# Turning the normalised softmax of a feed-forward: VectorE block transposes and DMA moves in place of TensorE transposes

## The chip, the cores and the metric

One NeuronCore of a Trainium2 chip runs the whole program. The metric is device time in microseconds. Three runs of the kernel before took 993.0, 997.02 and 998.18 us, with a median of 997.02 us.

## What is computed

The reference is a linear-attention recurrence over 768 time steps for 4 batches and 8 heads of 40 features, whose output is read as 3072 tokens of 320 features, followed by two feed-forward layers:

```python
h  = x @ w_in                                   # 320 -> 1024
sm = exp(h - max(h)) / (sum(exp(h - max(h))) + 1e-9)
solu = h * sm
ln = (solu - mean) / sqrt(var + 1e-6) * g_ln
x  = ln @ w_out                                 # 1024 -> 320
h2 = x @ w2_in                                  # 320 -> 2048
out = (max(h2, 0) + alpha * min(h2, 0)) @ w2_out  # 2048 -> 320
```

The change touches only the step between `ln` and `ln @ w_out` of the first feed-forward layer. The softmax, the mean and the variance run over the 1024 features of a token, so they are computed with tokens on the partitions; the product that follows contracts over the features, so its operand must have the features on the partitions. The normalised matrix is therefore turned (transposed) in between.

## The kernel before

**Stages.** The attention runs first, in 24 groups. The feed-forward is cut into 12 chunks of 256 tokens; a chunk has two tiles of 128 tokens (t = 0 and 1). Chunk 0's first layer runs beside the last attention groups. After that, `schedule` runs `step(c)` on each engine, c from 0 to 11 (steps 0 and 1 written out, steps 2 to 9 in a hardware loop over two at a time, steps 10 and 11 written out). Step c computes the second feed-forward layer of chunk c, and interleaved with it the first layer of chunk c + 1. So eleven of the twelve steps prepare a next chunk. Each engine runs its instructions strictly in the order in which the code lists them; semaphores connect the engines.

**TensorE in step c.** `layer1(c+1, 0)`, `layer2(c, 0)`, `layer1(c+1, 1)`, and then for q = 1 to 7 (each q is a pair of 128-feature blocks of the 2048) `layer2(c, q)` followed by `layer2_out(c, q-1)`. At q = 6, between the two, stand two calls of `turn_n`, one for each tile: 8 transposes of 128x128 each, from `soft[t]` into the PSUM tensor `bank`. After q = 7 come `layer1_out(c+1)`, which multiplies the turned matrix `nT` by `w_out` and needs both tiles (`nT_high`, `nT_low`), and `layer2_out(c, 7)`. All products are made of three matmuls of split operands: a high and a low part of each fp32 number.

**VectorE in step c.** `largest` (row maximum), `weigh` (the product h * sm), `normalise` (L1419, after a power that GpSimd computes) of chunk c + 1 are placed among the calls of `split(c, q)`, q = 0 to 7. `split` makes the rectified activation from `mid` and `slopes` (L1441), its high part (L1445) and its low part (L1368); `layer2_out(c, q)` on TensorE waits for it. `normalise(c+1, 0)` stands behind `split(c, 3)` and `normalise(c+1, 1)` behind `split(c, 4)`. `low_n` for both tiles (the low part of `nT`, L1368) stands behind `split(c, 6)`.

**ScalarE in step c.** `exponent` and `square` of chunk c + 1 among the calls of `rectify(c, q)` (L1278 and L1282), which make `slopes` from `mid`. `take_n` for both tiles (the high part of `nT`, rounded out of `bank`, L1222) stands behind `rectify(c, 6)`.

**SyncE in step c.** It issues all DMAs: three loads of x for chunk c + 2 (L1020), then it waits for `y_taken` and stores the output (L1087).

**Where a wait bites.** `layer2(c, q)` waits for `act_ready` of pair q - 2, `layer2_out(c, q)` waits for `act_low` of pair q. The buffer `stage2` (128x1024 fp32) serves as landing place for raw weights while step 0 runs, and is free after that. `soft[0]` and `soft[1]` are 128x1024 fp32 each.

Of the kernel before, what the change touches and what calls it, by code (L numbers as in the profile page):

```python
# [892 lines left out]
def feed_forward(nc, ctx, early, att, x_scr, wts, out):  # L893
# [53 lines left out]
    var_ready, rstd_ready, n_ready = sem("var_ready"), sem("rstd_ready"), sem("n_ready")  # L947
    nT_done, nT_high, nT_low = sem("nT_done"), sem("nT_high"), sem("nT_low")
    z_done, z_high, z_low = sem("z_done"), sem("z_high"), sem("z_low")
    z_part_ready, z_last_ready, z_last_high = sem("z_part_ready"), sem("z_last_ready"), sem("z_last_high")  # L950
# [37 lines left out]
    def wait_raw(eng, n):  # L988
        eng.wait_ge(raw_loaded[home[n]], 16 * len(held[n]) + 16)

    def bank(c, t):
        return banks[0 if isinstance(c, int) and c == 0 else t]
# [77 lines left out]
    def sync(sp):  # L1070
        sp.wait_ge(xT_low, 2)
        for n in range(7, len(pieces)):
            load_piece(sp, n)
        for saved in att["y_saved"]:
            sp.wait_ge(saved, NG // 2 * 16)
        sp.wait_ge(low_ready, len(pieces))

        def prologue():
            pass

        def step(c, k, nxt, far):
            if far:
                load_x(sp, c + 2, x_in[k])
            before = value(sp, c * 16)
            sp.wait_ge(y_taken, c * 2 + 2)
            wait(sp, y_saved, before)
            sp.dma_start(out[c], y_sb[:]).then_inc(y_saved, 16)  # L1087

        schedule(sp, prologue, step)
        sp.wait_ge(y_saved, NC * 16)  # L1090

    def tensor(pe):
# [6 lines left out]
        def layer1(c, t):  # L1099
# [8 lines left out]
            if isinstance(c, int) and c == 0 and t == 1:  # L1108
                pe.wait_ge(nT_high, 2)
                pe.wait_ge(nT_low, 1)  # L1110
# [11 lines left out]
        def turn_n(c, t):  # L1122

            pe.wait_ge(n_ready, 2 * c + t + 1)
            if isinstance(c, int) and c == 0 and t == 0:
                pe.wait_ge(small_loaded, 48)
# [5 lines left out]
        def layer1_out(c):  # L1132

            pe.wait_ge(nT_high, 4 * c + 4)
            pe.wait_ge(nT_low, 2 * c + 2)
# [64 lines left out]
        def step(c, k, nxt, far):  # L1200
# [5 lines left out]
            for q in range(1, PAIRS):  # L1206
                layer2(c, q)
                if nxt and q == 6:
                    for t in range(2):
                        turn_n(c + 1, t)  # L1210
                layer2_out(c, q - 1)
# [19 lines left out]
    def scalar(act):  # L1231
# [22 lines left out]
        def take_n(c, t):  # L1254

            if isinstance(c, int) and c == 0:
                act.wait_ge(att["rhs_done"], 21 + 2 * t)
            for half in range(2):
                act.wait_ge(nT_done, 4 * c + 2 * t + half + 1)
                high(act, nT[:, t, 0, half * 4:half * 4 + 4],  # L1260
                     bank(c, t)[:, half * 512:half * 512 + 512].rearrange("p (f t) -> p f t", f=4)).then_inc(nT_high, 1)

# [58 lines left out]
        def step(c, k, nxt, far):  # L1321
            if nxt:
                exponent(c + 1, 0)
            for q in range(PAIRS):
# [7 lines left out]
                if nxt and q == 3:  # L1332
                    square(c + 1, 1)
                if nxt and q == 6:
                    take_n(c + 1, 0)
                    take_n(c + 1, 1)
            if far:
# [38 lines left out]
    def vector(dve):  # L1376
# [45 lines left out]
        def low_n(c, t):  # L1422

            dve.wait_ge(nT_high, 4 * c + 2 * t + 2)
            if isinstance(c, int) and c == 0:
                dve.wait_ge(att["rhs_done"], 22 + 2 * t)
            low(dve, nT[:, t, 1], bank(c, t)[:].rearrange("p (f t) -> p f t", f=FT1), nT[:, t, 0]).then_inc(nT_low, 1)

# [69 lines left out]
        def step(c, k, nxt, far):  # L1498
            if nxt:
                largest(c + 1, 0)  # L1500
            for q in range(PAIRS):
# [9 lines left out]
                if nxt and q in (3, 4):  # L1511
                    normalise(c + 1, q - 3)
                if nxt and q == 6:
                    low_n(c + 1, 0)
                    low_n(c + 1, 1)
            if far:
# [112 lines left out]
```

## Time and profile before

| | value |
|---|---|
| median of three runs | 997.02 us (993.0 to 998.18) |
| profiled execution, first to last instruction (span) | 994.4 us |
| TensorE busy | 921.3 us, 93% of the span, 13248 matmuls |
| VectorE busy | 660.0 us, 66% |
| ScalarE busy | 437.6 us, 44% |
| GpSimd busy | 243.3 us, 24% |
| granted TensorE clock, mean | 0.972 |
| share of TensorE in the chain that ended last | 80% |

The page and the times give no total of the profiled execution's own beside its span; the median of the runs is 2.6 us above the span. The span has 31301 instructions. Busy time is an average over stages: the attention ends near 430 us, and the feed-forward's steps fill the rest. In a timeline a row tells the start in microseconds from the span's start, the duration, the engine, the line, the operation and what it writes and reads; what stands in brackets at its end is how long the engine was idle before it, and which instruction's end released it. "SPq" rows are DMA issues: the time that the sequencer spent on handing the transfer over, not the transfer. Successive instructions of one kind are merged into one row with a count.

### The profile page before, as it was taken

To read this page: it belongs to the slowest core of one execution; us is meant where nothing else is said; L and a number is where in the kernel's file an instruction comes from. 1 tells how busy PE (TensorE), PEld (TensorE's weight loads), DVE (VectorE), ACT (ScalarE), POOL (GpSimd) and SP (SyncE) were. 2 spreads that over 40 slices of the span, in tenths; PEclk is the share of its full clock that TensorE was granted. 3 is DMA by queue.
4 is the path that set the end of the run, shared out by engine and by line. 5 is a ranking of instruction groups with operands and counts; after the bars stand their busy time and mean duration, and the time that the engine had idled before them with its cause. 6 is when DMAs were issued, how large, how long until landed. Compare 5 with 4: busy or idle time off the path is not lost.

```text
span 994.4 us, 31301 instructions
## 1 busy us (share of the span) xinstructions
PE 921.3 (93%) x13248; PEld 874.5 (88%) x13248; DVE 660.0 (66%) x1135; ACT 437.6 (44%) x892; POOL 243.3 (24%) x453
## 2 busy tenths in 40 slices
PE   3378999999999989888999999999999999999997
PEld 3378989988999988887999999999999999999997
DVE  8967877878878655568565647575756656565734
ACT  3234444544545533346343535363434435353523
POOL 8676564765556550000000000000000000000000
PEclk9698999999999989989999999999999999999999
DMA  5725765557666542352011010000000000000000
GB/s 159 126 71 149 150 128 123 154 137 165 136 145 156 129 90 55 106 164 77 1 27 28 1 28 1 27 0 26 0 26 0 26 9 18 26 0 13 2 14 14
DMA packets 156813, 67.32 MB, mean 68 GB/s; under 512 B 120172, under 2 KB 146412, under 8 KB 156700
## 3 DMA queue, kind: packets, MB, share of 16 engines
q1 hardware_dynamic: 154588, 65.54, 27.6%
q8 instruction: 89, 1.46, 0.6%
q10 hardware_dynamic: 2112, 0.13, 0.2%
q14 instruction: 24, 0.20, 0.1%
HBM read 45.98 MB, written 19.66 MB: 66 GB/s over the span
## 4 chain that ended last, share of the span: by engine, by line
PE 80%; DVE 10%; issue 5%; ACT 3%; DMA 1%; POOL 1%; ACTq 0%; DVEq 0%; POOLq 0%
PE px L341 7%; PE acc L1095 6%; PE acc L1096 5%; PE acc L1097 5%; PE pq L402 5%; PE pa L310 4%; PE mid L1095 4%; PE mid L1096 4%; PE mid L1097 4%; PE bank L1095 3%; PE bank L1097 3%; PE bank L1096 3%; PE py L428 3%; PE pr L354 3%; PE pr L365 3%
## 5 line engine op out<-in xcount | busy, mean ns | idle before, releaser
L1354 POOL TENSOR_TENSOR stats<-stats 128x1 f32<-128x1 f32 x24 | 13.2, 549 | 552.8 <-DVE stats L1416 552.8
L1441 DVE SCALAR_TENSOR_TENSOR stage<-mid,slopes 128x512 f32<-128x512 f32 x96 | 66.4, 691 | 106.1 <-ACT slopes L1282 106.0
L1095 PE MATMUL acc<-wo_h,act_h 128*128 128x320 f32 x384 | 121.7, 317 | 8.4 <-DVE act_l L1368 7.7
L1278 ACT ACTIVATE stage<-mid 128x512 f32<-128x512 f32 x96 | 57.1, 595 | 160.2 <-PE mid L1166 160.2
L1096 PE MATMUL acc<-wo_h,act_l 128*128 128x320 f32 x384 | 118.5, 309 | 0.0
L1097 PE MATMUL acc<-wo_l,act_h 128*128 128x320 f32 x384 | 118.2, 308 | 0.0
L1095 PE MATMUL mid<-zT_h,w_h 128*128 128x256 f32 x384 | 107.9, 281 | 2.3 <-DVE zT_l L1368 2.3
L1096 PE MATMUL mid<-zT_h,w_l 128*128 128x256 f32 x384 | 107.5, 280 | 0.0
L1097 PE MATMUL mid<-zT_l,w_h 128*128 128x256 f32 x384 | 107.3, 279 | 0.0
L793 POOL TENSOR_TENSOR al<-al,prod 40x512 f32<-40x512 f32 x48 | 70.7, 1473 | 97.9 <-DMA al<-a_features_first 85.5
L1282 ACT ACTIVATE slopes<-stage,minus_alpha 128x256 f32<-128x256 f32 x192 | 87.3, 502 | 3.1
L1095 PEld LDWEIGHTS acc<-wo_h,act_h 128*128 128x128 f32 x384 | 72.2, 188 | 13.0 <-issue 11.0
L1095 PEld LDWEIGHTS mid<-zT_h,w_h 128*128 128x128 f32 x384 | 72.8, 190 | 3.5 <-DVE zT_l L1368 2.7
L1096 PEld LDWEIGHTS mid<-zT_h,w_l 128*128 128x128 f32 x384 | 72.8, 190 | 0.8
L1097 PEld LDWEIGHTS mid<-zT_l,w_h 128*128 128x128 f32 x384 | 72.9, 190 | 0.0
L1096 PEld LDWEIGHTS acc<-wo_h,act_l 128*128 128x128 f32 x384 | 72.4, 188 | 0.0
L1097 PEld LDWEIGHTS acc<-wo_l,act_h 128*128 128x128 f32 x384 | 72.2, 188 | 0.0
L310 PE MATMUL pa<-a_bd,wkb 128*128 128x128 f32 x336 | 54.8, 315 | 18.2 <-ACT a_bd L708 11.1
L1368 DVE TENSOR_TENSOR act_l<-stage,act_h 128x512 fp32r<-128x512 f32 x96 | 66.5, 692 | 3.3
L310 PEld LDWEIGHTS pa<-a_bd,wkb 128*128 128x128 f32 x336 | 46.9, 217 | 20.3 <-DMA masks<-masks_in 11.0
L816 POOL TENSOR_TENSOR s_x<-s_x,s_t 128x15 f32<-128x15 f32 (+4 forms) x165 | 61.3, 372 | 12.9
L1245 ACT ACTIVATE soft<-bank,stats 128x1024 f32<-128x1024 f32 x24 | 26.6, 1108 | 74.1 <-DVE stats L1399 74.1
(162 smaller groups left out, 2410.0 us busy)
## 6 DMA issues: line engine op xcount, KB each, us to landing
wkb<-wkb_features_first SPq DMA_DIRECT2D x46, 242.5 KB
rvu<-rv_features_first SPq DMA_DIRECT2D x48, 160.0 KB
l_scr<-lb SPq DMA_DIRECT2D x24, 256.0 KB, 4.4
x_scr<-x SPq DMA_DIRECT2D x24, 256.0 KB, 3.7
al<-a_features_first SPq DMA_DIRECT2D x48, 80.0 KB
sv<-v_time_first SPq DMA_DIRECT2D x48, 80.0 KB, 4.7
out<-y_sb SPq DMA_DIRECT2D x12, 320.0 KB, 2.2
d_scr<-s_x SPq DMA_DIRECT2D x12, 256.0 KB, 2.3
```

Source lines behind the costliest of these rows:

```text
L310: ins = pe.matmul(banks[:, h * P:(h + 1) * P], kbT[m % 3][:, h].rearrange("p a b -> p (a b)"), a_bd[:, :, h], start=True, stop=True)
L341: ins = pe.matmul(px[half * HALF:half * HALF + rows, h * T + first:(h + 1) * T], left, right, start=True, stop=True)
L402: ins = pe.matmul(pq[:, h * P:(h + 1) * P], vuT[m % 3][:, h].rearrange("p a b -> p (a b)"), rvu[m % 3][:, h, 0:4:3], start=True, stop=True)
L793: pool.tensor_tensor(al[m % 7][r, half], al[m % 7][r, half], prod[m % 9][r, :, 0:T], ALU.mult)\
L816: link(pool.tensor_tensor(tgt, tgt, s_t[:, 0:n_t, 0:n_j], ALU.subtract))
L1095: pe.matmul(o, left[0], right[0], start=start, stop=False)
L1096: pe.matmul(o, left[1], right[0], start=False, stop=False)
L1097: return pe.matmul(o, left[0], right[1], start=False, stop=stop)
L1278: act.activation(neg[q % 2][:], mid[q % 2][:], ACT.Relu, scale=-1.0).then_inc(neg_ready, 1)
L1282: act.activation(slope[q % 2][:, cols], neg[q % 2][:, cols], ACT.Copy, scale=minus_alpha[:, 2 * q + f:2 * q + f + 1]).then_inc(slope_ready, 1)
L1368: return dve.tensor_tensor(out_, in_, hi.bitcast(F32), ALU.subtract)
L1441: dve.scalar_tensor_tensor(out=act_f[q % 2][:], in0=mid[q % 2][:], scalar=0.0, in1=slope[q % 2][:], op0=ALU.max, op1=ALU.add).then_inc(act ...
```

## The change

From chunk 1 on, the turning of the normalised matrix takes another path; chunk 0 keeps the old one.

- TensorE no longer turns in the steps (the two calls of `turn_n` at q = 6 are gone).
- VectorE gets a `turn_n` of its own, right behind each `normalise`: one transpose instruction on 128x1024 fp32 that transposes every 32x32 block inside its own group of 32 partitions, from `soft[t]` into `turned` (the buffer `stage2`, one for both tiles). Before it, it waits on `n_moved` until the moves of the tile before have landed, since `turned` is single.
- SyncE gets `move_n`: per tile 16 DMAs, each of 32 partitions x 256 fp32 numbers (32 KB), which carry each block from `turned` to the partitions where it belongs, back into `soft[t]`. Each tile's 16 DMAs raise `n_moved` by 256. They stand behind the loads of x of the same step and in front of the store of the output.
- ScalarE's `take_n` is one instruction per tile in place of two, reads `soft[t]` in place of `bank`, and waits for `n_moved` of its tile. It moves from behind `rectify(c, 6)` (both tiles) to behind `rectify(c, 5)` (tile 0) and `rectify(c, 6)` (tile 1).
- VectorE's `low_n` reads `soft[t]` and moves likewise: behind `split(c, 5)` for tile 0 and behind `split(c, 6)` for tile 1.

```diff
--- before.py
+++ after.py
@@ -946,6 +946,7 @@
     soft_ready, mean_ready, square_ready = sem("soft_ready"), sem("mean_ready"), sem("square_ready")
     var_ready, rstd_ready, n_ready = sem("var_ready"), sem("rstd_ready"), sem("n_ready")
     nT_done, nT_high, nT_low = sem("nT_done"), sem("nT_high"), sem("nT_low")
+    tr_ready, n_moved = sem("tr_ready"), sem("n_moved")
     z_done, z_high, z_low = sem("z_done"), sem("z_high"), sem("z_low")
     z_part_ready, z_last_ready, z_last_high = sem("z_part_ready"), sem("z_last_ready"), sem("z_last_high")
     mid_done, act_ready, act_high, act_low = sem("mid_done"), sem("act_ready"), sem("act_high"), sem("act_low")
@@ -987,6 +988,18 @@
 
     def wait_raw(eng, n):
         eng.wait_ge(raw_loaded[home[n]], 16 * len(held[n]) + 16)
+
+    turned = stage2
+
+    def token_blocks(z):
+
+        return z.rearrange("p f (i t) -> p f i t", i=4)
+
+    def moved_n(c, t):
+
+        if isinstance(c, int) and c == 0:
+            return bank(c, t)[:].rearrange("p (f i t) -> p f i t", f=FT1, i=4)
+        return soft[t][:].rearrange("p (i f t) -> p f i t", i=4, f=FT1)
 
     def bank(c, t):
         return banks[0 if isinstance(c, int) and c == 0 else t]
@@ -1078,9 +1091,20 @@
         def prologue():
             pass
 
+        def move_n(c, t):
+
+            sp.wait_ge(tr_ready, 2 * c + t - 1)
+            for q in range(4):
+                for i in range(4):
+                    sp.dma_start(soft[t][32 * q:32 * q + 32, i * 256:i * 256 + 256],
+                                 turned[32 * i:32 * i + 32, q * 256:q * 256 + 256]).then_inc(n_moved, 16)
+
         def step(c, k, nxt, far):
             if far:
                 load_x(sp, c + 2, x_in[k])
+            if nxt:
+                for t in range(2):
+                    move_n(c + 1, t)
             before = value(sp, c * 16)
             sp.wait_ge(y_taken, c * 2 + 2)
             wait(sp, y_saved, before)
@@ -1106,7 +1130,7 @@
                 pe.wait_ge(w1_low, KT)
                 pe.wait_ge(att["kbn_ready"], 2 * NG)
             if isinstance(c, int) and c == 0 and t == 1:
-                pe.wait_ge(nT_high, 2)
+                pe.wait_ge(nT_high, 1)
                 pe.wait_ge(nT_low, 1)
             tok = slice(t * P, (t + 1) * P)
             for half in range(2):
@@ -1121,8 +1145,8 @@
 
         def turn_n(c, t):
 
-            pe.wait_ge(n_ready, 2 * c + t + 1)
-            if isinstance(c, int) and c == 0 and t == 0:
+            pe.wait_ge(n_ready, t + 1)
+            if t == 0:
                 pe.wait_ge(small_loaded, 48)
             for f in range(FT1):
                 ins = pe.transpose(bank(c, t)[:, f * P:(f + 1) * P], soft[t][:, f * P:(f + 1) * P], ident[:])
@@ -1131,7 +1155,7 @@
 
         def layer1_out(c):
 
-            pe.wait_ge(nT_high, 4 * c + 4)
+            pe.wait_ge(nT_high, 2 * c + 2)
             pe.wait_ge(nT_low, 2 * c + 2)
             def both(z):
                 return z.rearrange("p (t k) -> p t k", t=2)
@@ -1205,9 +1229,6 @@
                 layer1(c + 1, 1)
             for q in range(1, PAIRS):
                 layer2(c, q)
-                if nxt and q == 6:
-                    for t in range(2):
-                        turn_n(c + 1, t)
                 layer2_out(c, q - 1)
             if nxt:
                 layer1_out(c + 1)
@@ -1255,10 +1276,10 @@
 
             if isinstance(c, int) and c == 0:
                 act.wait_ge(att["rhs_done"], 21 + 2 * t)
-            for half in range(2):
-                act.wait_ge(nT_done, 4 * c + 2 * t + half + 1)
-                high(act, nT[:, t, 0, half * 4:half * 4 + 4],
-                     bank(c, t)[:, half * 512:half * 512 + 512].rearrange("p (f t) -> p f t", f=4)).then_inc(nT_high, 1)
+                act.wait_ge(nT_done, 2 * t + 2)
+            else:
+                act.wait_ge(n_moved, (2 * c + t - 1) * 256)
+            high(act, token_blocks(nT[:, t, 0]), moved_n(c, t)).then_inc(nT_high, 1)
 
         def take_z(c):
 
@@ -1331,9 +1352,8 @@
                     exponent(c + 1, 1)
                 if nxt and q == 3:
                     square(c + 1, 1)
-                if nxt and q == 6:
-                    take_n(c + 1, 0)
-                    take_n(c + 1, 1)
+                if nxt and q in (5, 6):
+                    take_n(c + 1, q - 5)
             if far:
                 take_x(act, c + 2, x_in[k])
             if nxt:
@@ -1421,10 +1441,17 @@
 
         def low_n(c, t):
 
-            dve.wait_ge(nT_high, 4 * c + 2 * t + 2)
+            dve.wait_ge(nT_high, 2 * c + t + 1)
             if isinstance(c, int) and c == 0:
                 dve.wait_ge(att["rhs_done"], 22 + 2 * t)
-            low(dve, nT[:, t, 1], bank(c, t)[:].rearrange("p (f t) -> p f t", f=FT1), nT[:, t, 0]).then_inc(nT_low, 1)
+            low(dve, token_blocks(nT[:, t, 1]), moved_n(c, t), token_blocks(nT[:, t, 0])).then_inc(nT_low, 1)
+
+        def turn_n(c, t):
+
+            dve.wait_ge(n_ready, 2 * c + t + 1)
+            wait(dve, n_moved, (2 * c + t - 2) * 256)
+            dve.transpose(turned[:].rearrange("p (q f t) -> p q f t", q=4, f=FT1),
+                          soft[t][:].rearrange("p (f q r) -> p q f r", q=4, f=FT1)).then_inc(tr_ready, 1)
 
         def low_z(c):
 
@@ -1510,9 +1537,9 @@
                     weigh(c + 1, 1)
                 if nxt and q in (3, 4):
                     normalise(c + 1, q - 3)
-                if nxt and q == 6:
-                    low_n(c + 1, 0)
-                    low_n(c + 1, 1)
+                    turn_n(c + 1, q - 3)
+                if nxt and q in (5, 6):
+                    low_n(c + 1, q - 5)
             if far:
                 low_x(dve, c + 2, x_in[k])
             if nxt:
```

## Rows read from the trace of the kernel before

**Rows 1.** Windows: stretch, length; busy of PE, PEld, DVE, ACT, POOL; clock; DMA; GB/s.

```profile
664.00:705.00 41.00, 40.72 (x298) 39.07 (x297) 24.65 (x46) 18.74 (x38) 0.55 (x1) 1.00 0.06 16
```

**Rows 2.** The waits, TensorE from 470 us on: total us, times, longest.

```profile
PE acc L1095 <- DVE act_l L1368: 6.4, 11, 1.8
```

**Rows 3.** The chain that ended last, from 440 us on, in one step.

```profile
663.65 1.75 PE bank L1128 x16
...
709.64 1.75 PE bank L1128 x16
...
716.73 1.84 PE bank L1142 x16
```

**Rows 4.** TensorE's timeline in that step.

```profile
705.89 0.31 PE L1095 MATMUL acc<-wo_h,act_h 128*128 128x320 f32 x1
...
707.65 0.28 PE L1095 MATMUL mid<-zT_h,w_h 128*128 128x256 f32 x1
...
709.47 1.91 PE L1128 MATMUL bank<-ident,soft 128*128 128x128 f32 x16
...
711.14 0.39 PE L1095 MATMUL acc<-wo_h,act_h 128*128 128x320 f32 x1
```

**Rows 5.** VectorE's timeline in the same step.

```profile
702.75 0.81 DVE L1419 TENSOR_SCALAR soft<-soft,stats 128x1024 f32<-128x1024 f32 x1 [0.66 <-POOL stats L1354]
...
703.73 0.69 DVE L1441 SCALAR_TENSOR_TENSOR stage<-mid,slopes 128x512 f32<-128x512 f32 x1 [0.17 <-ACT slopes L1282]
...
704.92 0.69 DVE L1368 TENSOR_TENSOR act_l<-stage,act_h 128x512 fp32r<-128x512 f32 x1
...
706.35 0.81 DVE L1419 TENSOR_SCALAR soft<-soft,stats 128x1024 f32<-128x1024 f32 x1 [0.67 <-POOL stats L1354]
...
713.04 2.35 DVE L1368 TENSOR_TENSOR nT<-bank,nT 128x1024 fp32r<-128x1024 f32 x2
...
725.87 0.89 DVE L1454 COPY y_sb<-acc 128x320 f32<-128x320 f32 x2 [0.50 <-PE acc L1097]
```

**Rows 6.** ScalarE's timeline in the same step.

```profile
709.67 0.60 ACT L1278 ACTIVATE stage<-mid 128x512 f32<-128x512 f32 x1 [2.04 <-PE mid L1166]
...
710.30 0.91 ACT L1282 ACTIVATE slopes<-stage,minus_alpha 128x256 f32<-128x256 f32 x2
```

**Rows 7.** SyncE's timeline: DMA issues at three places.

```profile
48.71 0.71 SPq L185 DMA_DIRECT2D al<-a_features_first  x2
...
49.46 0.71 SPq L178 DMA_DIRECT2D wkb<-wkb_features_first  x2
...
315.81 5.26 SPq L232 DMA_DIRECT2D dd<-d_scr  x8
...
726.93 0.37 SPq L1087 DMA_DIRECT2D out<-y_sb  x1
```

**Rows 8.** DMA issues: KB each, median us from issue to landing.

```profile
out<-y_sb SPq DMA_DIRECT2D x12, 320.0 KB, 2.2
...
dd<-d_scr SPq DMA_DIRECT2D x92, 32.0 KB, 3.0
...
d_scr<-s_x SPq DMA_DIRECT2D x12, 256.0 KB, 2.3
```

**Rows 9.** Groups by line and form, 560 to 900 us: busy us, mean ns.

```profile
L1419 DVE TENSOR_SCALAR soft<-soft,stats 128x1024 f32<-128x1024 f32 x16 | 13.0, 813 | 10.6 <-POOL stats L1354 10.6
...
L1251 ACT ACTIVATE bank<-soft,stats 128x1024 f32<-128x1024 f32 x15 | 16.5, 1100 | 0.0
```

**Rows 10.** TensorE's timeline in the last step.

```profile
961.20 0.39 PE L1095 MATMUL acc<-wo_h,act_h 128*128 128x320 f32 x1 [1.82 <-DVE act_l L1368]
```

**Rows 11.** One-microsecond stretches of the last step, columns as in rows 1.

```profile
960.00:961.00 1.00, 0.00 (x0) 0.00 (x0) 0.97 (x3) 0.91 (x3) 0.00 (x0) 1.00 0.00 0
...
964.00:965.00 1.00, 1.00 (x7) 1.00 (x7) 0.00 (x0) 0.00 (x0) 0.00 (x0) 0.50 0.00 0
...
966.00:967.00 1.00, 1.00 (x10) 1.00 (x9) 0.00 (x0) 0.36 (x1) 0.00 (x0) 1.00 0.00 0
```

## The prediction

> **What bounds the kernel now.** I read the windows first. A stretch of 41 us in the middle of the steps has TensorE busy for 40.72 us at a granted clock of 1.00, VectorE for 24.65, ScalarE for 18.74, and the DMA engines 0.06 [rows 1]. So TensorE sets the pace, and the other engines and the DMA have time to spare on average. The waits say the same: from 470 us on, TensorE waited 6.4 us for another engine, 11 times [rows 2]. The chain of waits then gives the period: the turning of one step starts at 663.65 and that of the next at 709.64, 45.99 us apart [rows 3]. Last come the timelines of one step, and they show what the averages hide. VectorE and ScalarE run at a short distance ahead of TensorE. The low part of pair 4 is ready at 704.92 + 0.69 = 705.61 [rows 5], and TensorE starts on it at 705.89 [rows 4]: 0.28 us of slack. The question is therefore not how busy VectorE is, but how long a thing stands in front of a `split`.
>
> **What is removed.** Per step, TensorE's 16 transposes stand between 709.47 and 711.14 [rows 4], 1.67 us by this, 1.75 by the chain [rows 3]. Nothing overlaps them on TensorE, so they are on the path: 11 steps x 1.75 = 19.3 us, if nothing takes their place.
>
> **VectorE's transpose, T.** No transpose of VectorE is in this trace. The nearest rows for 1024 fp32 numbers a partition are 0.81 us (one input, SBUF to SBUF, L1419) [rows 9] and 2.35 / 2 = 1.175 us (L1368) [rows 5]. I take T = 1.2, at the slower one, since every number has to pass the rearrangement. Bounds: 0.81 and twice the slower row, 2.4. The Trainium skill, VectorE: DVE Perf Modes, "The three transpose paths", gives 311 ns for a 128x128 block of bf16, and 8 of these would be 2.5 us as an estimate, with a start-up counted 8 times; no row here shows one, and with 2.5 the sum below would be 29 us longer.
>
> **The moves, D.** Per tile SyncE issues 16 DMAs one after the other. An issue isn't free: two DMAs of 40 rows each take 0.71 us together, four in a row from 48.71 end at 50.17, so 0.365 each; a single one in the quiet steps takes 0.37; the eight DMAs of `dd`, also 32 KB but cut into far smaller pieces, take 5.26, 0.66 each [rows 7]. Ours have 32 rows of one piece of 1 KB, which is nearest to the 40 rows, and the queue is otherwise quiet. I take 0.37. Landing: 2.2 and 2.3 us for transfers out of SBUF, 3.0 for `dd` [rows 8]; I take 2.2. From the end of an instruction of VectorE to SyncE's issue that waits for it: 725.87 + 0.89 = 726.76 to 726.93 [rows 5, 7], 0.17. So D = 0.17 + 15 x 0.37 + 2.2 = 7.9 us from the end of a transpose to the last landing. Bounds: 0.17 + 15 x 0.33 + 1.7 = 6.8 (a tenth and half a microsecond off) and 0.17 + 15 x 0.66 + 3.0 = 13.1. The Trainium skill speaks the other way in DMA: Bandwidth & Descriptors, "Issuing engines are not separate DMA queues": the sequencer's time to start a DMA is usually small beside the DMA itself. The rows disagree for a transfer of this size: 16 issues are 5.9 us, a landing 2.2.
>
> **What queues behind what.** `turned` is single, so VectorE's second transpose waits for the first tile's moves, and `split(c, 5)`, which TensorE needs, stands behind it. ScalarE's `take_n` waits for the moves with `rectify` behind it. Take the step of the rows:
>
> - `normalise` of tile 0 ends at 702.75 + 0.81 = 703.56 [rows 5]. Transpose to 704.76. Its moves land at 704.76 + 7.9 = 712.7.
> - `split(4)` runs from 704.76 instead of 703.73 and takes 705.61 - 703.73 = 1.88 [rows 5]: ready 706.64, so TensorE starts on pair 4 some 0.9 us later than at 705.89. `normalise` of tile 1 is done by 708.3 (from 705.61 to 706.35 + 0.81 is 1.55 us [rows 5]).
> - The second transpose can't start before 712.7, and ends at 713.9. `split(5)` ends at 715.8, and TensorE starts `layer2_out(5)` at 715.9, where it was 711.14 [rows 4]. `layer2(6)` ended near 706.8 + 1.76 + 1.82 = 710.4, so TensorE has been idle for 5.5 us.
> - The moves of tile 1 land at 713.9 + 7.9 = 721.8. ScalarE's single `take_n` costs 1.1 (L1251, same size [rows 9]): 722.9. `low_n` costs 1.2 [rows 5]: 724.1. TensorE reacts by 724.2.
> - Meanwhile TensorE does pair 5, `layer2(7)` and pair 6, 1.76 + 1.82 + 1.76 = 5.3 us (707.65 - 705.89 and 709.47 - 707.65 [rows 4]), until 721.3. Pair 6 is ready in time: `rectify(6)` (0.60 + 0.91 [rows 6]) starts behind `take_n` of tile 0 at 713.8, and `split(6)` behind `low_n` of tile 0 at 717.0 ends at 718.9. TensorE then waits a second time, 2.9 us, for `layer1_out`.
> - `layer1_out` starts at 724.2 where it was 716.73 [rows 3]: **7.5 us later per step**, the 1.75 saved already counted. `rectify(7)` and `split(7)`, held up by `take_n`, end near 726.5, under the 64 products of `layer1_out` (16 of them take 1.84 us [rows 3], so 7.4 in all). What follows is as before.
>
> **Clock.** A stall costs more than itself if the clock falls. In the last step, TensorE waits 1.82 us before 961.20 [rows 10]; the granted clock was 1.00 in that gap, 0.50 (1.2 GHz) in 964 to 965 and 1.00 (2.4 GHz) again in 966 to 967 [rows 11]. So up to 5 us at half clock followed, 2.4 us of work lost, at least 0.5. Here the first gap is longer, so I expect half clock behind 715.9; but the work from there has 2.9 us to spare before `layer1_out`, which covers it. What the second, shorter gap then brings I put at 0.4 us a step.
>
> **The sum.** 11 x (7.5 + 0.4) = 87 us. Span 994.4 + 87 = 1081. The median of the runs is 2.6 us above the span, so the time is **1084 us**. The formula behind it, per step: 2D + 2T + 1.1 + 1.2 + 0.1 - (716.73 - 703.56) = 2D + 2T - 10.8.
>
> The other edits come to nothing: the shorter wait list of `layer1`, one ScalarE instruction for two, and `low_n` on SBUF in place of PSUM. SyncE has nothing else due; the store of the output is behind the moves but waits for a later event anyway, and its next loads of x are needed a step later.
>
> **Rivals.**
>
> - *Issuing at the slow pace.* If back-to-back DMAs pile up as those of `dd` do, D = 13.1: 2 x 5.2 x 11 = 114 us more, 1198. Halfway, 0.5 us an issue, D = 9.9: 44 us more, 1128. Against it: the eight of `dd` have many small pieces each.
> - *A slow transpose.* T = 2.4: 2 x 1.2 x 11 = 26 us more, 1110. The trace says nothing against it.
> - *The clock isn't covered.* If half clock outlasts the slack or falls again in `layer1_out`, up to 2.4 us a step: 22 us more, 1106.
> - *The other side: the moves are hidden and the change pays.* This decides at D: by the formula nothing is lost through `layer1_out` when 2D + 2T is 10.8, so D = 4.2 with T = 1.2, and the second transpose isn't held up if D is at most 3.5. Then T alone counts. With T = 0.81, `split(4)` ends at 706.25 and the second transpose at 708.6, `split(5)` at 710.5, and TensorE is at pair 5 at 710.6 in place of 711.14: 11 x 0.5 = 5.5 us gained, 991. With T = 1.2, TensorE is there at 711.5, 0.3 later: 1001. So even hidden moves give back most of the 19.3 us, for the two transposes stand in front of two `split`s that had hardly any slack. For it: a time by bytes would be short, as 320 KB land in 2.2 us [rows 8]. Against it: no row shows an issue much under 0.36 us. The Trainium skill's rule on issue time, in the section named above, would lead here.
> - *It doesn't do what it says.* That the turning stays on TensorE is excluded by the code; no chance is left for it.
>
> **How the numbers follow.** Forecast (D 6.8 to 8.7, T up to 1.5): 0.58, its own range 1060 to 1108. Slow issue: 0.17. Slow transpose: 0.11. Clock: 0.08. Hidden moves: 0.06, half of it with a fast transpose. The low end is D = 6.8: 11 x 2 x 1.1 = 24 us less, 1060, with a little for smaller T: 1056. The high end takes in the slow transpose and the halfway issue, 1128, and the two in part together: 1145. A measurement here can tell some 0.5%, 5 us, from no change. Faster by more than that: 0.03; within: 0.03; slower: 0.94.
>
> **What would show it.** Right: SyncE's timeline has blocks of 16 DMAs, 5.9 us long, two a step; TensorE's waits name `act_l` with 5 to 6 us and `nT` with 1 to 3 us, 11 times each; the period between two `layer1_out` is near 53.9 us; VectorE's second transpose waits for a DMA. The prediction is wrong if the issue takes less than 0.3 us or more than 0.45, if a transpose takes over 1.5 us, or if the granted clock stays at 0.50 for much of a step.

## The result, and the profile after

The changed kernel takes 1188.44 us in the median of 4 runs (1182.24 to 1193.2), the kernel before 995.01 (991.11 to 998.18) beside it: a ratio of 1.193, 95% interval 1.187 to 1.198. The profiled execution took 1182.24 us, its span is 1180.5. That is 186.1 us above the span of before. The predicted time was 1084, in a range of 1056 to 1145: the direction and the chain of waits were right, but the slow-down forecast was 87 us and the one measured 193, outside the range. Ratios are taken from fast runs alone; a run more than 1.5% above the fastest of its kernel is not among them.

The page shows where to look: TensorE's share of the span falls from 93% to 81%, and a new kind of DMA stands first in the list of issues.

```profile
PE 953.6 (81%) x13072; PEld 900.5 (76%) x13072; DVE 682.9 (58%) x1157; ACT 436.6 (37%) x868; POOL 241.3 (20%) x453
...
soft<-stage SPq DMA_DIRECT2D x352, 32.0 KB, 1.8
```

The waits of TensorE from 470 us on (total us, times, longest), which answer to [rows 2]: 6.4 us have become 159.5.

```profile
PE acc L1119 <- DVE act_l L1388: 112.5, 33, 9.8
PE bank L1166 <- DVE nT L1388: 47.0, 11, 4.8
```

VectorE's timeline in one step, which answers to [rows 5] (there `normalise` of tile 0 starts at 702.75, here at 724.58):

```profile
724.58 0.81 DVE L1439 TENSOR_SCALAR soft<-soft,stats 128x1024 f32<-128x1024 f32 x1 [0.66 <-POOL stats L1374]
725.52 1.25 DVE L1453 STREAM_TRANSPOSE stage<-soft 128x1024 f32<-128x1024 f32 x1
...
738.13 1.25 DVE L1453 STREAM_TRANSPOSE stage<-soft 128x1024 f32<-128x1024 f32 x1 [8.06 <-DMA soft<-stage]
739.30 0.65 DVE L1468 SCALAR_TENSOR_TENSOR stage<-mid,slopes 128x512 f32<-128x512 f32 x1
...
751.80 1.23 DVE L1388 TENSOR_TENSOR nT<-soft,nT 128x1024 fp32r<-128x1024 f32 x1 [7.73 <-ACT nT L1243]
```

SyncE's and ScalarE's in the same step, and TensorE's, which answer to [rows 7, 6, 4]:

```profile
726.79 22.63 SPq L1099 DMA_DIRECT2D soft<-stage  x32
```

```profile
750.71 1.06 ACT L1243 ACTIVATE nT<-soft 128x1024 fp32r<-128x1024 f32 x1 [10.09 <-DMA soft<-stage]
```

```profile
741.29 0.60 PE L1119 MATMUL acc<-wo_h,act_h 128*128 128x320 f32 x1 [8.73 <-DVE act_l L1388]
...
753.17 3.75 PE L1166 MATMUL bank<-nT,wo_h 128*128 128x256 f32 x16 [4.61 <-DVE nT L1388]
```

Read them in order. The first transpose ends at 726.77 and SyncE issues sixteen DMAs. VectorE has been idle for 8.06 us when they have landed and its second transpose starts; `split(5)` stands behind it, and TensorE waits 8.73 us. Then SyncE issues the other sixteen (its row merges both blocks; the 22.63 us hold a break of 2.5 us between them), `take_n` waits until they have landed, with ScalarE idle for 10.09 us, and TensorE waits 4.61 us in front of `layer1_out`. The first 16 products of `layer1_out` take 3.75 us; TensorE's timeline of before has them at 716.57, in 2.00 us (the chain of [rows 3], which measures to the next start, says 1.84 from 716.73). One-microsecond stretches of the same step (columns as in rows 1) show why:

```profile
743.00:744.00 1.00, 1.00 (x5) 1.00 (x5) 0.97 (x2) 0.00 (x0) 0.00 (x0) 0.50 0.26 66
745.00:746.00 1.00, 1.00 (x11) 1.00 (x10) 0.00 (x0) 0.00 (x0) 0.00 (x0) 1.00 0.26 66
...
754.00:755.00 1.00, 1.00 (x6) 1.00 (x6) 0.97 (x2) 0.02 (x1) 0.00 (x0) 0.50 0.00 0
759.00:760.00 1.00, 1.00 (x11) 1.00 (x10) 0.00 (x0) 0.00 (x0) 0.00 (x0) 1.00 0.00 0
```

The granted clock is 0.50 (1.2 GHz) behind the first gap until about 745, as long as pair 5 runs, and again behind the second gap until between 758 and 759, in `layer1_out`.

The account of a step, read from the timelines of all eleven steps that prepare a next chunk. From the end of `normalise` of tile 0 to the start of `layer1_out` it takes 27.95 us on average (27.78 in the step shown), before 13.01: 14.9 us more. The formula of the prediction, 2D + 2T - 10.8, gives 14.5 with what the rows now show: D = 738.13 - 726.77 = 11.4 for both tiles, T = 1.25. `layer1_out` itself, up to the next product, takes 9.43 us on average where it took 7.28, 2.15 more; that is the clock. The rest of a step is the same, 25.7 us in both. 11 x (14.9 + 2.15) = 188 us; the spans differ by 186.1, since what lies outside these steps is 2 us shorter in this profile.

So two terms of the sum were too small: D (7.9 taken) and the clock (0.4 taken). By the spans, 1180.5 in place of 1081, 99 us were missed (104 by the medians). D is the large one, 11 x 2 x 3.5 = 77 us; the clock is 11 x 1.75 = 19.

### The profile page after: what moved, and what is told of

It reads as the page before. It is cut to its first block, busy times and chain, and to the rows that moved or that the text cites. A ratio compares the mean times of both kernels' runs of the same rounds, so it can differ in the third digit from the quotient of the medians.

```text
span 1180.5 us, 31280 instructions
## 1 busy us (share of the span) xinstructions
PE 953.6 (81%) x13072; PEld 900.5 (76%) x13072; DVE 682.9 (58%) x1157; ACT 436.6 (37%) x868; POOL 241.3 (20%) x453
## 4 chain that ended last, share of the span: by engine, by line
issue 46%; PE 15%; POOL 13%; SPq 10%; DMA 9%; DVE 5%; ACT 2%; POOLq 0%; DVEq 0%; ACTq 0%
SPq L232 5%; POOL s_x L816 5%; POOL s_t L814 5%; SPq L1099 5%; DMA d_scr<-s_x 3%; DMA s_in<-l_scr 2%; POOL al L793 1%; DMA al<-a_features_first 1%; PE bank L1119 1%; PE bank L1120 1%; PE bank L1121 1%; PE px L341 1%; DMA soft<-stage 1%; POOL s_x L809 1%; PE bank L1166 1%
## 5 line engine op out<-in xcount | busy, mean ns | idle before, releaser
L1119 PE MATMUL acc<-wo_h,act_h 128*128 128x320 f32 x384 | 130.4, 340 | 114.3 <-DVE act_l L1388 113.7
L1120 PE MATMUL acc<-wo_h,act_l 128*128 128x320 f32 x384 | 125.9, 328 | 0.0
L1121 PE MATMUL acc<-wo_l,act_h 128*128 128x320 f32 x384 | 125.6, 327 | 0.0
L1243 ACT ACTIVATE nT<-soft 128x1024 fp32r<-128x1024 f32 x22 | 23.2, 1056 | 208.7 <-DMA soft<-stage 208.7
L1166 PE MATMUL bank<-nT,wo_h 128*128 128x256 f32 x192 | 42.1, 404 | 49.5 <-DVE nT L1388 49.5
L1453 DVE STREAM_TRANSPOSE stage<-soft 128x1024 f32<-128x1024 f32 x22 | 27.4, 1245 | 90.9 <-DMA soft<-stage 89.7
L1166 PEld LDWEIGHTS bank<-nT,wo_h 128*128 128x128 f32 x192 | 39.3, 309 | 52.2 <-issue 52.2
L1120 PEld LDWEIGHTS acc<-wo_h,act_l 128*128 128x128 f32 x384 | 78.9, 205 | 0.0
L1121 PEld LDWEIGHTS acc<-wo_l,act_h 128*128 128x128 f32 x384 | 78.8, 205 | 0.0
L1388 DVE TENSOR_TENSOR nT<-soft,nT 128x1024 fp32r<-128x1024 f32 x22 | 26.9, 1222 | 86.2 <-ACT nT L1243 86.2
```

The lines of the kernel that those rows point to most:

```text
L1119: pe.matmul(o, left[0], right[0], start=start, stop=False)
L1120: pe.matmul(o, left[1], right[0], start=False, stop=False)
L1121: return pe.matmul(o, left[0], right[1], start=False, stop=stop)
L1166: ins = pe.matmul(o, wo1[0][:, f, 2 * P:DP], nT[:, :, part, f], start=f == 0 and part == 0, stop=f == FT1 - 1 and part == 1)
```

## The experiments

The edits below are shortened to the lines that matter; two dots in a line stand for what is unchanged.

### Taking TensorE's transposes away alone

```diff
-  act.wait_ge(n_moved, (2 * c + t - 1) * 256)
+  act.wait_ge(n_ready, 2 * c + t + 1)
```

(with the moves and VectorE's `turn_n` emptied). Expected:

> From the changed kernel, VectorE's transpose and the moves are left out and nothing turns the matrix from chunk 1 on (the high and low parts are taken from the unturned matrix, so the output is not the reference's). It is the most that taking TensorE's transposes away can give. My theory, that the low part of pair 5 is ready at 709.54 in the step of the trace of before, so TensorE can start on it at 709.7 in place of 711.14: 11 x 1.45 = 16 us less than before, 979. Rival, that all of the 1.75 us a step is given back: 19 us, 976. Rival, that the distance between the engines is tighter than the rows say: 990.

Measured: 977.33 us against 994.01, ratio 0.982 (0.974 to 0.989), 16.7 us less. The interval, 11 to 26 us, can't tell this from 19.3. The trace can: from one `layer1_out` to the next it is 44.5 us in the steps that repeat, where it was 46.0. So the most that this idea can give, with everything else free, is 1.5 us a step and not the 1.75 that TensorE's own rows show, because the low part of pair 5 is ready only just in time (at 702.26, and TensorE starts on it at 702.40).

### VectorE's transposes alone, on top of the kernel before

```diff
   normalise(c + 1, q - 3)
+  turn_extra(c + 1, q - 3)   # dve.transpose(turned, soft[t]), read by nobody
```

> The kernel before with one thing added: VectorE's transpose behind each normalise, its result read by nobody; TensorE still turns, no moves. My theory: 1.245 us stand in front of split(4), which has 0.28 us of slack, so TensorE starts on pair 4 about 0.95 us later in each of 11 steps: 10 us more than before, 1005. The second transpose costs nothing beyond, as TensorE's own turning stands in front of pair 5. Rival: VectorE is busy 60% of a step, so 2.5 us more a step are absorbed: 995.

Measured: 1007.37 us against 994.01, ratio 1.013 (1.006 to 1.020), 13.4 us more. TensorE's timeline shows the place:

```profile
707.84 0.39 PE L1097 MATMUL acc<-wo_h,act_h 128*128 128x320 f32 x1 [0.76 <-DVE act_l L1370]
```

TensorE's waits for `act_l`, from 470 us to the end, are 13.5 us in 21 cases, where they were 6.4 in 11 [rows 2]. VectorE is 60% busy, and 2.5 us a step more of it still cost about 1.2 us a step (47.0 us from one `layer1_out` to the next, and 3 us more in the first step), for the place is in front of a `split` that had 0.28 us to spare. With e1 this says: even moves that take no time would leave at most 3 us of the gain. And e2 doesn't price the second transpose, which TensorE's own turning hides there; once that turning is gone, `split(5)` has no time to spare either.

### What makes an issue 0.59 us long

Each kernel here is the changed one with another form of the moves; all waits stay. The groups of SyncE's line in the changed kernel and in two of them (duration ns min/median/max of an issue):

```profile
L1099 SPq DMA_DIRECT2D soft<-stage x352: 507/591/1453, 473.1 to 1126.7; - x176
```

```profile
L1099 SPq DMA_DIRECT2D soft<-w_out x352: 310/421/1397, 474.2 to 1060.9; - x176
```

```profile
L1099 SPq DMA_DIRECT2D t_scr<-stage x352: 302/421/1855, 471.5 to 1051.3; - x176
```

**Source in DRAM** (second fence):

```diff
-   turned[32 * i:32 * i + 32, q * 256:q * 256 + 256]
+   wts["w_out"][32 * i:32 * i + 32, q, 0:256]
```

> The changed kernel with the source of the 16 moves taken from DRAM (parts of w_out of the same shape, 32 rows of 1 KB, so the output is not the reference's) in place of the buffer turned; all waits stay. Theory A, that an issue takes 0.59 us instead of 0.37 because both sides are in SBUF: issues of 0.37, the block of 32 issues about 15 us in place of 22.6, 11 x 2 x 15 x 0.22 = 73 us less than the changed kernel, 1115, less what DRAM costs in landing. Theory B, that the issue's time hangs on the form of the transfer (rows, pieces) or on something else that stays: 0.59, 1188.

Measured: 1117.47 us, 71 less than the changed kernel. The block of 32 issues takes 17.17 us in place of 22.63 and D is 8.8. Neither 0.37 nor 0.59 but 0.42 an issue; the time fits since the second gap shrinks too (2.1 us on average, where it was 4.3). One care with these figures: 0.42 and 0.59 are the time of one issue alone, and 0.04 us lie between two, so start to start they are 0.46 and 0.63, to be compared with the 0.365 of [rows 7]. The sides account for 0.17 of the 0.27 by which the prediction missed; the 0.10 between its 40-row transfers and these 32-row ones, both out of DRAM, isn't explained.

**Destination in DRAM** (third fence):

```diff
-   sp.dma_start(soft[t][32 * q:32 * q + 32, i * 256:i * 256 + 256],
+   sp.dma_start(wts["t_scr"][t, 32 * q:32 * q + 32, i * 256:i * 256 + 256],
```

> The changed kernel with the 16 moves of a tile going from turned to DRAM and not back into soft (so the output is not the reference's); counts, rows and waits stay. With the source in DRAM an issue took 0.42 us (block of 32 in 17.2 us), with both sides in SBUF 0.59. Theory A, that it is both sides being in SBUF together: about 0.42 here too, D near 8.8, 1115. Theory B, that it is the source in SBUF: 0.59, 1185.

Measured: 0.42 us an issue again, 1104.01 in a single run, with landings of 1.6 us in place of 1.8. So it is not the source: with one side in DRAM, whichever, an issue of this shape is 0.42 us, with both sides in SBUF 0.59 (the median of 352 issues in each of the three traces).

**Half of each row:**

```diff
-  soft[t][.., i * 256:i * 256 + 256], turned[.., q * 256:q * 256 + 256]
+  soft[t][.., i * 256:i * 256 + 128], turned[.., q * 256:q * 256 + 128]
```

> The changed kernel with half of each row moved (128 in place of 256 numbers, so the output is not the reference's). Theory, that an issue's 0.59 us don't depend on bytes: 1188 as before, at most 3 us less. Rival, that the sequencer is held up by the transfer itself (a full queue): issues near 0.37 and 1115.

Measured: 1182.28 us, median issue 0.591, landing 1.8. Halving the bytes changes neither.

**No change of partitions:** `turned[32 * q:32 * q + 32, i * 256:...]` as the source.

> The changed kernel with each block taken from the partitions where it goes (no move from one group of 32 to another, so the output is not the reference's). Theory, that both sides in SBUF make the issue 0.59 us long, whatever the partitions: 1188. Rival, that going from one group of partitions to another makes it long: 0.37 an issue, 1115.

Measured: 1186.34 us, median issue 0.591. Going from one group of partitions to another plays no part.

**4 DMAs of 128 rows in place of 16 of 32:**

```diff
-  for q in range(4):
-      for i in range(4):
-          sp.dma_start(soft[t][32*q:32*q+32, i*256:i*256+256], turned[32*i:32*i+32, q*256:q*256+256])
+  for i in range(4):
+      sp.dma_start(soft[t][:, i*256:i*256+256], turned[:, i*256:i*256+256])
```

> The changed kernel with 4 moves of 128 rows of 1 KB a tile in place of 16 of 32 rows: the same bytes, each part on its own partitions, so the output is not the reference's. Theory, that the issue's time goes by the DMA and not by its rows: 4 issues of about 0.6, D = 0.1 + 3 x 0.6 + 2.2 = 4.1, by my formula 2D + 2T - 10.8 about 0 a step, and what is left is VectorE's transposes in front of the splits: 995 to 1002. Rival, that it goes by rows: 2.4 us an issue, 1188.

Measured: 1013.83 us, ratio 1.020 (1.013 to 1.026). An issue takes 0.60 us, D falls to 4.0 us with the same 512 KB a tile, and both sides are still in SBUF: so the price goes by the number of DMAs, and this run is the cleanest evidence for it. The time is 12 us above what I expected: two steps had single moves 2 us longer, and the period is 47.0 us where the prediction's 0.3 us a step for hidden moves gives 46.3. The transpose still waits 0.65 us for the moves here (its row: `[0.65 <-DMA soft<-stage]` at 721.67), in front of `split(5)`, on top of its own 1.25; that makes up the difference.

### The clock

**Filling TensorE's gaps with short transposes.** The changed kernel and, with results read by nobody:

```diff
+  if nxt and q == 6: fill(c + 1, 72)   # pe.transpose(bank[:, 0:P], ident, ident)
   layer2_out(c, q - 1)
 ...
+  fill(c + 1, 32)
   layer1_out(c + 1)
```

> The changed kernel with work added: 72 transposes of the identity on TensorE in front of layer2_out(5) (7.5 us, in a gap of 9) and 32 in front of layer1_out (3.3 us in a gap of 4.6), results read by nobody. If the fall of the granted clock costs 3 us in each layer1_out, as its first 16 products (3.75 us instead of 1.84) say, the clock stays at 1.00 and the kernel gets 11 x 3 = 33 us faster than the changed one: 1155. If the slow layer1_out has another cause (its operands, the DMA writes), it stays at 1188 or gets slower by what the added work overhangs: 1190 to 1200.

Measured: 1189.74 us, no change. In the step looked at the clock stayed at 1.00 through pair 5, but the second filling ended 3.4 us before `layer1_out`, and its stretch at 757 to 758 is at 0.50; over the eleven steps `layer1_out` still took 9.1 us. So I made that filling longer, 64:

> As e3_busy_pe, with 64 in place of 32 transposes in front of layer1_out. In e3_busy_pe the first gap was filled and the granted clock stayed at 1.00 through pair 5 to pair 6, but the filling in front of layer1_out ended at 751.7 and layer1_out began at 755.2, and the clock fell to 0.50 behind that gap of 3.5 us. 64 transposes (6.7 us) leave about 0.3 us. Theory that the clock makes layer1_out slow: clock 1.00 in it, 11 x 3 = 33 us less than the changed kernel, 1156. Rival, that layer1_out is slow for another reason behind the moves: 1189.

Measured: 1183.77 us (1178.08 to 1189.14), a miss. The mean granted clock is 1.00 from 470 to 1120 us, and `layer1_out` takes 7.45 us on average, 2.0 less than in the changed kernel, yet the total hardly moves. In the profiled execution the 2.0 us come back in two places. The moves had become longer, by up to 1.3 us a tile in most of the steps, so `layer1_out` starts 29.3 us behind `normalise` in place of 27.95. And the rest of a step grew from 25.7 to 26.5 us, in part by three gaps of 1.7 to 2.1 us, two steps apart, in which TensorE waited for no other engine (at 706.8, 833.5 and 961.8). Queue 8, which carries the instruction loads (packets, MB, share), from 520 to 990 us, in the changed kernel, in this one, and in the next:

```profile
q8 instruction: 7, 0.11, 0.1%
```

```profile
q8 instruction: 35, 0.57, 0.6%
```

```profile
q8 instruction: 8, 0.13, 0.1%
```

**Few long instructions as filling.** 9 and 7 plain fp32 products of 128x512 in place of 72 and 64 transposes:

> As e3b_busy_longer, with few long instructions as filling: 9 and 7 plain fp32 products of 128x512 in place of 72 and 64 short transposes. In e3b_busy_longer the granted clock was 1.00 from 470 us on and layer1_out took its full-clock time, 10.3 us from take_n to take_z in place of 12.1, but the moves had got up to 1 us a tile longer, and the queue of instruction loads carried 35 packets in a stretch where the changed kernel's carried 7: the longer loop body is loaded again and again. If that is what gave the gain back, the moves take 11.4 us a tile again here and the time is the changed kernel's less 11 x 1.75 = 19 us: 1169. Rival, that a busy TensorE itself makes the issues longer: moves up to 12.4 us, 1184.

Measured: 1167.85 us (1165.81 to 1169.0), ratio to before 1.174. That is 20.6 us less than the changed kernel, by adding work to its busiest engine. In the stretch from 470 to 1150 us the clock is 1.00 where the changed kernel had 0.88, the moves take 11.4 us in 9 of the 11 steps' first tiles, and the rest of a step is 25.7 us again. So the clock cost about 20 us, 1.9 a step. The instruction loads are the likely reason for e3b's longer moves and gaps: the packets and the moves went up and down together (e3 itself had 31 packets and longer moves). That a load holds up SyncE's issue is not shown beyond that.

**Not every gap brought the slow clock.** In the last step of most of these kernels TensorE waits the same 1.8 us in front of a product. The granted clock fell to 0.50 behind it for some 3.4 us in the kernel before, the changed kernel, e9 and e12; in e1, e2, e3b and e3c it stayed at 1.00. In e12 eleven gaps of 2.3 to 3.1 us stand in front of `layer1_out`, and the clock fell behind one of them. One of those that left it alone (the sixteen products take 2.12 us):

```profile
732.75 2.12 PE L1165 MATMUL bank<-nT,wo_h 128*128 128x256 f32 x16 [2.32 <-DVE nT L1390]
```

Behind the changed kernel's gaps of 3.8 us and more in front of `layer1_out` it fell every time. In e3 gaps of 3.4 and 3.5 us at the same place went either way. What decides it in the shorter ones is open.

### Two buffers in place of one

```diff
-  turned = stage2
+  turned = [stage2, late_stage]      # late_stage made 64 bytes longer
-  wait(dve, n_moved, (2 * c + t - 2) * 256)
+  wait(dve, n_moved[t], (c - 1) * 256)
```

> The changed kernel with a buffer turned for each tile, so VectorE's second transpose no longer waits for the first tile's moves; still 16 DMAs a tile on one queue. If the issues alone set the end, the second block follows the first at once: 31 x 0.6 + 1.9 = 20.5 us from the first issue to the last landing, in place of 24.0: 11 x 3.5 = 38 us less, 1150, and up to 10 us of it given back by the clock behind a longer second gap. Rival, that the wait for the buffer is the main cost (it holds VectorE for 8 us a step): 1188 - 11 x 8 = 1100.

Measured: 1161.65 us, 27 less than the changed kernel. VectorE's second transpose no longer waits, and 32 issues follow each other without a break:

```profile
719.90 10.07 SPq L1098 DMA_DIRECT2D soft<-stage  x16
730.02 10.10 SPq L1098 DMA_DIRECT2D soft<-late_stage  x16
```

The rival is out: freeing VectorE from a wait of 8 us a step gives 2.4 (1.8 by the spans of the profiled executions), for the second tile's moves only queue behind the first tile's. The start of `layer1_out` moves 2.5 us forward; the clock gives 0.7 of it back, as `layer1_out` takes 10.1 us in place of 9.4.

### Five DMAs a tile in place of sixteen

```diff
-  for q in range(4):
-      for i in range(4):
-          sp.dma_start(soft[t][32*q:32*q+32, i*256:i*256+256], turned[32*i:32*i+32, q*256:q*256+256])
+  sp.dma_start(wts["t_scr"][t], turned[:]).then_inc(n_out, 16)
+  sp.wait_ge(n_out, (2 * c + t - 1) * 16)
+  for q in range(4):
+      sp.dma_start(soft[t][32*q:32*q+32].rearrange("r (i x) -> r i x", i=4),
+                   wts["t_scr"][t][:, q*256:q*256+256].rearrange("(i r) x -> r i x", i=4))
```

> The changed kernel with 5 DMAs a tile in place of 16: one writes all of turned to DRAM, and behind its landing four read it back, 32 partitions each. My account of the change by the number of issues: D = 0.2 + 0.4 + 2.2 for the write and 0.1 + 3 x 0.45 + 2.5 for the reads = 6.7 in place of 11.4, so 2 x 4.7 = 9.4 us a step less, 103 in all: 1085; and shorter gaps leave the clock up, some 10 us less still: 1070 to 1085. Rival, that the moves are bound by bytes or landings, which double here: 1188 or more.

Measured: 1066.68 us, ratio to before 1.071 (1.066 to 1.076): 122 us less than the changed kernel, with twice the bytes moved and two landings in a row. SyncE's timeline of one step:

```profile
687.36 0.36 SPq L1097 DMA_DIRECT2D t_scr<-stage  x1
690.01 1.76 SPq L1100 DMA_DIRECT2D soft<-t_scr  x4
```

D is 7.1. This turns the whole matrix as the changed kernel does. It changes two things at once, the number of DMAs and the sides (each has one side in DRAM), so it confirms the price of the issues as a whole; e7 separates the number, e4 and e11 the sides.

### One tile only, and nothing in front of a tight wait

Tile 1 stays on TensorE. `normalise` of tile 0 goes behind `split(1)`, where VectorE has 1.6 us free, its transpose behind `split(3)`, and both `take_n` and `low_n` stay behind `rectify(6)` and `split(6)`. The moves are the five DMAs over DRAM.

```diff
-  if nxt and q in (3, 4):
-      normalise(c + 1, q - 3)
-      turn_n(c + 1, q - 3)
+  if nxt and q in (1, 4):
+      normalise(c + 1, q // 4)
+  if nxt and q == 3:
+      turn_n(c + 1, 0)
```

> Only tile 0 is turned by VectorE and DMA (over DRAM, 5 DMAs), tile 1 by TensorE as before. normalise of tile 0 moves up behind split(1), where VectorE has 1.6 us free, its transpose stands behind split(3), take_n and low_n of both tiles stay behind rectify(6) and split(6). By the rows of before the transpose ends at 703.2, the moves land at 709.9, and take_n is due at 711.2: hidden by 1.3 us. No split starts later than before. TensorE loses 8 of 16 transposes, 0.87 us: 11 x 0.87 = 9.6 us less than before, 984, ratio 0.990. Rival, that the moves aren't hidden (take_n waits, 1 us or more a step): 995 to 1010.

Measured: 986.95 us in the median of six runs (979.81 to 1001.43) against 995.15 (989.15 to 998.64). The ratio of 0.988 (0.984 to 0.992) is of four of the six; the two longest, 994.89 and 1001.43, are not in it, the medians of all runs stand at 0.992, and the ranges overlap. So the times alone make a gain of about 1% likely and not certain. The trace is firmer: from one `layer1_out` to the next it is 45.13 us in place of 45.99 in the steps that repeat, the 0.87 expected. It is the one variant that turns all of the matrix and isn't slower than the kernel before. In its timeline ScalarE takes the moved tile without a wait, and TensorE has 8 transposes left:

```profile
709.66 1.05 ACT L1246 ACTIVATE nT<-soft 128x1024 fp32r<-128x1024 f32 x1
```

```profile
708.01 1.04 PE L1153 MATMUL bank<-ident,soft 128*128 128x128 f32 x8
```

**The same with the sixteen direct moves:**

> As e9_one_tile, with the 16 direct moves in place of the 5 DMAs over DRAM. By the trace of e9_one_tile the transpose of tile 0 ends 8.0 us before its take_n is due, and 9.1 us before rectify(6) is done; with 11.4 us for the moves take_n starts 3.4 us later than due, and the low parts and layer1_out follow; VectorE had 1.8 us to spare there. So 11 x (3.4 - 1.8) = 18 us more than e9_one_tile: 1005, slower than before by 1%. Rival, that the direct moves are hidden when only one tile goes that way (half the issues): 987.

Measured: 1024.62 us, ratio 1.029 (1.023 to 1.036). One edit turns the gain into a loss:

```profile
729.15 1.06 ACT L1244 ACTIVATE nT<-soft 128x1024 fp32r<-128x1024 f32 x1 [3.36 <-DMA soft<-stage]
```

The 3.4 us that `take_n` is late were right, the 1.8 us of slack behind it were not: in e9's rows the last `low_n` ends at 713.9 and `layer1_out` starts 0.3 us later. TensorE waits 28.0 us for `nT` in 11 steps, 2.5 each. The step is 47.9 us against 45.1 in most cases, up to 49.5 in two, and the first is 3 us longer as well; this adds up to all of the 33 us between the two profiled spans. The medians differ by 37.7; the 5 us beyond are in the spread of the runs (1019.44 to 1031.08 here) and aren't explained.

## Why the prediction was wrong, and what of it was right

- **The gain, 19.3 us.** It was counted as if all of it could be had; by e1's trace 1.5 us a step, 16.5 in all, were there.
- **T, 1.2 us.** Right: 1.245. The Trainium skill, VectorE: DVE Perf Modes, "The three transpose paths", by which an estimate of 2.5 stood beside the sum, gives 311 ns for 128x128 in bf16. The row shows 1245 ns for 8 times as many columns in fp32, 4 times the page's figure and not 8. A start-up counted once would fit, but no run has a smaller transpose that would show it.
- **The chain.** Right: the second transpose behind the first tile's moves, `split(5)` behind it, `take_n` behind the second moves, `low_n`, `layer1_out`. With the measured D and T its formula gives 14.5 us a step, and 14.9 were measured. The small items were right as well (0.17 to SyncE; 1.06 for `take_n`, 1.1 taken; 1.23 for `low_n`, 1.2 taken).
- **D, 7.9 us: the step that failed.** "Ours have 32 rows of one piece of 1 KB, which is nearest to the 40 rows" took the issue from transfers out of DRAM, 0.37 us. The likeness in rows and pieces was the wrong one; most of the difference is that both sides lie in SBUF here (0.17 us an issue, by e4 and e11), and 0.10 is open. Counted start to start, as the 0.37 was, an issue took 0.63. The landing was taken too long, 2.2 for 1.8. D = 0.1 + 15 x 0.63 + 1.8 = 11.4. The sign that the prediction had set for itself, an issue of more than 0.45, was there. Of its rivals the one of the slow pace was the nearer, with 0.66 us an issue and 1198 us, though its D of 13.1 was too long by the landing and its reason, many small pieces, was another one. The forecast's range was closed below it, and slow issues had 0.17 in all.
- **The clock, 0.4 us a step.** Mis-sized: about 2. I let the 2.9 us of slack behind the first gap cover all of it. The first gap's half clock was indeed covered, though that gap was 8.7 us and not 5.5, for `layer1_out` waits for the moves anyway. But the second gap was 4.3 us on average and not 2.9, and it brought its own, in `layer1_out`, where nothing covers it. That the 0.4 was low is therefore in part a consequence of D. The one case that the prediction had, [rows 10, 11] (1.8 us idle, half clock from about 962.5 to 966), was thin ground for either number, since the same gap left the clock alone in four other traces.
- **The rival on the other side.** Its threshold for `layer1_out`, D under 4.2, was borne out: with D = 4.0 (e7) TensorE doesn't wait for `nT` in ten of the eleven steps, and the kernel is 2% slower and not 19%. That nearly hidden moves still give back the whole gain is what e7 and e2 show.
- The Trainium skill's rule in DMA: Bandwidth & Descriptors, "Issuing engines are not separate DMA queues", that starting a DMA takes little beside the DMA itself, doesn't help for 32 KB here: of the 1.8 us from issue to landing the issue is 0.59, and sixteen of them are 16 x 0.63 = 10 us. It holds for one DMA of 512 KB: 0.36 us of issuing, 2.6 to the landing (e8).

## What to carry to other kernels

Count the DMAs, not the bytes: a chain of small DMAs on one queue costs its issues one after the other, and whatever waits for the last of them waits for all. Moving work from the bounding engine to one with spare time pays only where it stands in front of nothing that the bounding engine needs soon; read the slack at that place from the timeline, not the busy share. And price each gap of TensorE with the clock behind it, at the place where the slow stretch will lie, as a range: here the same gap cost nothing in one trace and a stretch of 3.4 us at half clock in another.

## What the runs showed of the hardware

- A DMA issue from SyncE of 32 rows by 1 KB takes 0.59 us when both sides lie in SBUF, 0.42 when one side is in DRAM (either one), with 0.04 between two; half the bytes or the same partitions on both sides don't change the first, and 128 rows take 0.60. One DMA of 128 rows by 4 KB from SBUF to DRAM takes 0.36 (e8).
- VectorE's transpose of 128x1024 fp32 in 32x32 blocks takes 1.245 us, about as long as the subtraction of that size behind it (`low_n`, 1.22).
- In the changed kernel, behind gaps of 3.8 to 9.8 us, TensorE ran at half clock for some 3 to 6 us of work. Behind gaps of 1.8 to 3.5 us the clock fell in some traces and not in others. Kept busy with products whose results nobody reads, it stayed at 1.00 on average, and the kernel got 20.6 us faster (e3c).
- Adding 136 short transposes to each step of the loop raised the instruction loads from 7 to 35 packets in 470 us, the DMA issues beside them got slower, and TensorE had gaps of its own; 16 long products for the same time didn't (8 packets).
